# Six units of 512 tokens instead of eight of 384 in a fused attention and two-layer kernel, with the second result kept feature-major

## What is computed

```python
for t in range(S):
    state = alpha[:, :, t, :, None] * state + einsum('bhd,bhe->bhde', k[:, :, t], v[:, :, t])
    y[:, :, t] = einsum('bhd,bhde->bhe', q[:, :, t], state)
```

## Time and profile before

| quantity | value |
|---|---|
| median of 3 runs | 1025.24 us (1024.99 to 1027.24) |
| profiled execution, span | 1023.4 us |
| PE busy | 999.5 us, 98% |
| DVE, ACT, POOL busy | 399.3, 464.0, 81.0 us |
| mean granted PE clock | 0.997 of 2.4 GHz |
| instructions in the span | 16903 |

### The profile page before, as it was taken

How to read it: one execution, slowest core, us unless ns; L and a number is a source line. 1 busy time by engine, 2 the same in 40 slices (tenths; PEclk the granted TensorE clock), 3 DMA queues, 4 the chain that set the end, 5 groups by cost and what they waited for, 6 DMA issues and landing times.

```text
span 1023.4 us, 16903 instructions
## 1 busy us (share of the span) xinstructions
PE 999.5 (98%) x6146; PEld 950.8 (93%) x6146; DVE 399.3 (39%) x805; ACT 464.0 (45%) x1017; POOL 81.0 (8%) x110
## 2 busy tenths in 40 slices
PE   5989999999999999999999999999999999999997
PEld 5788898998898998998989999999999999999997
DVE  6583563562563743743732451212121212221211
ACT  4464563553543643634634774333333333343432
POOL 4663300000000000000000430000000000000000
PEclk9999999999999999999999999999999999999999
DMA  7661340230320321222000531010000000000000
GB/s 169 159 143 49 77 101 13 61 68 18 77 47 18 76 47 38 58 49 44 25 7 18 161 113 37 11 37 21 26 22 25 23 23 24 23 25 21 23 0 26
DMA packets 118465, 51.21 MB, mean 50 GB/s; under 512 B 103040, under 2 KB 115328, under 8 KB 118400
## 3 DMA queue, kind: packets, MB, share of 16 engines
q1 hardware_dynamic: 114304, 37.76, 15.5%
q0 software_dynamic: 4096, 12.59, 3.9%
HBM read 36.18 MB, written 9.44 MB: 45 GB/s over the span
## 4 chain that ended last, share of the span: by engine, by line
PE 95%; DVE 2%; issue 1%; ACT 1%; DMA 1%; SPq 0%; POOL 0%; DVEq 0%; ACTq 0%
PE z_ps L557 40%; PE h_ps L544 39%; PE job_ps L514 4%; PE job_ps L528 3%; PE job_ps L494 3%; PE job_ps L524 3%; PE job_ps L507 2%; PE job_ps L499 1%; DVE qp L814 1%; DVE rcp L819 0%; ACT L717 0%; DMA nat_a<-in_alpha 0%; DMA x_raw<-y_sb 0%; PE h_ps L586 0%; DVE kp L827 0%
## 5 line engine op out<-in xcount | busy, mean ns | idle before, releaser
L884 DVE TENSOR_TENSOR g_lo<-g,g_hi 128x384 fp32r<-128x384 f32 x256 | 141.2, 552 | 573.4 <-ACT g_hi L720 322.3
L544 PE MATMUL h_ps<-x_hi,win_hi 128*128 128x384 f32 x768 | 259.8, 338 | 4.7 <-issue 1.6
L544 PE MATMUL h_ps<-x_hi,win_lo 128*128 128x384 f32 x768 | 258.4, 336 | 0.0
L544 PE MATMUL h_ps<-x_lo,win_hi 128*128 128x384 f32 x768 | 258.4, 336 | 0.0
L717 ACT ACTIVATE g<-h_ps 128x384 f32<-128x384 f32 x128 | 62.9, 492 | 221.7 <-PE h_ps L544 221.6
L723 ACT ACTIVATE relu<-h_ps 128x384 f32<-128x384 f32 x128 | 62.7, 490 | 218.2 <-PE h_ps L544 213.5
L544 PEld LDWEIGHTS h_ps<-x_hi,win_hi 128*128 128x128 f32 x768 | 144.1, 188 | 6.5 <-ACT g L717 2.0
L544 PEld LDWEIGHTS h_ps<-x_lo,win_hi 128*128 128x128 f32 x768 | 144.1, 188 | 0.0
L544 PEld LDWEIGHTS h_ps<-x_hi,win_lo 128*128 128x128 f32 x768 | 144.1, 188 | 0.0
L557 PE MATMUL z_ps<-g_hi,wout_hi 128*128 128x384 f32 x384 | 138.0, 359 | 0.0
L557 PE MATMUL z_ps<-g_hi,wout_lo 128*128 128x384 f32 x384 | 129.5, 337 | 0.0
(11 more groups left out here) (68 smaller groups left out, 1016.7 us busy)
## 6 DMA issues: line engine op xcount, KB each, us to landing
w_raw<-in_moe_w_in POOLq DMA_DIRECT2D x32, 192.0 KB, 3.0
w_raw<-in_moe_w_out POOLq DMA_DIRECT2D x32, 192.0 KB, 2.7
nat_a<-in_alpha SPq DMA_DIRECT2D x24, 192.0 KB, 3.4
nat_k<-in_k SPq DMA_DIRECT2D x24, 192.0 KB, 3.5
nat_q<-in_q SPq DMA_DIRECT2D x24, 192.0 KB, 3.8
v_sb<-in_v SPq DMA_DIRECT2D x24, 192.0 KB, 3.8
z_scratch<-z_sb SPq DMA_DIRECT2D x24, 192.0 KB, 1.9
x_raw<-z_scratch SPq DMA_DIRECT2D x8, 576.0 KB, 4.0
```

The source lines that it names most:

```text
L544: last = nc.tensor.matmul(h_ps[f % 2][:, 0:UT], w[:, f, tile(kk)], x[par][:, kk, :], start=(kk == 0 and n == 0), stop=(kk == KD - 1 and n ...
L884: nc.vector.tensor_tensor(g_lo[s % 3][:], g[s % 2][:], g_hi[s % 3][:].bitcast(F32), ALU.subtract).then_inc(g_lo_made, 1)
```

## The change

The time axis is cut differently. A unit is one chunk of 128 tokens of all four batches: 6 units (UNITS = SEQ // P) of UT = 512 tokens. The products of both layers then have 512 columns; there are 6 x 16 x 18 of them in a layer instead of 8 x 16 x 18.

- The steps of both layers form one line of 192 (F), written out without loops, and the second product is two steps behind the first also across units and from layer one to layer two.
- The second layer's second product has w_out as weights, as the first layer's. Its result is feature-major in PSUM; DVE turns it in blocks of 32x32 (`turn_z`), and w_out's columns are permuted when they are split so that a row of a token's result lies in runs of 96 floats. A unit is stored by 16 DMAs of 48 KB with runs of 384 bytes; those of the last unit are shared by SP and ACT.
- The attention works on 24 pair units n (unit n // 4, pair n % 4; four tiles, one of each batch) in stages: A, KQ, S (scores of both heads, and KT), I, Y. Stages of n = 0 to 3, and A of n = 4, run ahead of everything (AHEAD). Those of n = 4 to 7 take three steps a pair, from n = 8 on four steps a pair. The last four pair units have no KT and I. A is no longer copied by ACT: DVE's scan reads PSUM. nat, kp, qp and v are kept for two pairs, not for a unit.
- Loads bring one head of one pair unit (96 KB) instead of one chunk of all heads (192 KB). 20 chunks of weights are split ahead of the first step instead of 16, five to a pair. The `relu` tile is gone; g is squared in place.

```diff
-UT = 384
-NC = UT // P
-UNITS = TOK // UT
+UNITS = SEQ // P
+UT = BATCH * P
+AHEAD = [("A", 0), ("A", 1), ("KQ", 0), ("S", 0), ("A", 2), ("KQ", 1), ("I", 0), ("Y", 0), ("S", 1), ("A", 3),
+         ("KQ", 2), ("I", 1), ("Y", 1), ("S", 2), ("KQ", 3), ("I", 2), ("Y", 2), ("S", 3), ("I", 3), ("Y", 3), ("A", 4)]
+FIRST_PE = {0: 6, 1: 8, 2: 8, 3: 4}
+WARM_AFTER = 24
+EARLY_CHUNKS = 20
+def stage_step(kind, n):
+    if n < 2 * PAIRS:
+        return {"A": -1, "KQ": 1, "S": 2, "I": 3, "Y": 3}[kind] + 3 * (n - PAIRS)
+    return {"A": -21, "KQ": -19, "S": -18, "I": -17, "Y": -16}[kind] + 4 * n
+    # within a step: S, A, I, Y, KQ
...
 # PE
+            def a_stage(n):
+                loaded("a", n)
+                if n > PAIRS:
+                    if has_state(n - 1):
+                        wait(pe, kt_copied, n)
...
+            def kq_stage(n):
...
+                turn("k", n, job_ps[0]).then_inc(k_made, 1)
+                loaded("q", n)
+                if n > PAIRS and has_state(n - 1):
+                    wait(pe, inc_made, 2 * n)
+                else:
+                    wait(pe, masked, 2 * n - 1)
+                turn("q", n, job_ps[1]).then_inc(q_made, 1)
+            def s_stage(n):
+                wait(pe, k_scaled, n + 1)
+                wait(pe, q_scaled, n + 1)
+                wait(pe, y_copied, n)
+                for b in range(BATCH):
+                    for h in (0, 1):
+                        r = head_rows(h)
+                        last = nc.tensor.matmul(job_ps[1 + h][:, tile(b)], kp[n % 2][r, tile(b)], qp[n % 2][r, tile(b)],
                                                 start=True, stop=True)
...
+            def y_stage(n):
...
+                    for b in range(BATCH):
+                        nc.tensor.matmul(ps[0:ROWS, tile(b)], state[:, p, b, :], qp[n % 2][:, tile(b)],
+                                         start=(b == 0), stop=False, skip_group_check=True)
+                for b in range(BATCH):
+                    for h in (0, 1):
+                        last = nc.tensor.matmul(ps[head_rows(h), tile(b)], v_sb[n % 2][:, b, h, :], score[h][:, b, :],
...
             def first_product(u, par, f, w_hi, w_lo):
                 wait(pe, act_made, NF * u + f - 1)
...
+            for F in range(2 * STEPS + LAG):
+                u, f = divmod(F, NF)
...
+                        first_product(u, u % 2, f, win_hi, win_lo)
+                    for kind, n in beside(F):
+                        stage(kind, n)
...
 # ACT
+            for n in range(PAIRS):
+                bounds(n)
+                for c in range(5 * n, 5 * n + 3):
+                    split_chunk(c)
+                kt_copy(n)
+                for c in range(5 * n + 3, 5 * n + 5):
+                    split_chunk(c)
+                y_copy(n)
+            split_x(0, ys=1)
+            bounds(PAIRS)
+            for F in range(2 * STEPS):
+                u, f = divmod(F, NF)
+                step(u, f, F % 3, u >= UNITS)
+                if u < UNITS:
+                    square_g(f)
+                if u == 0 and EARLY_CHUNKS + f < NCHUNK:
+                    split_chunk(EARLY_CHUNKS + f)
...
+                if f == 1 and 1 <= u <= UNITS:
+                    copy_z(u - 1, u - 1, u - 1)
+                for kind, n in beside(F):
+                    if kind == "S" and has_state(n):
+                        kt_copy(n)
+                    if kind == "Y":
+                        y_copy(n)
+                for kind, n in beside(F - 1):
+                    if kind == "A":
+                        bounds(n)
...
 # DVE
+            def a_stage(n):
+                at, ps = qp[n % 2], a_bank(n)
...
+                for b in range(BATCH):
+                    nc.vector.tensor_tensor_scan(out=at[:, tile(b)], data0=ps[0:ROWS, tile(b)], data1=floor[:],
...
+                for half in (0, 1):
+                    cols = slice(half * UT // 2, (half + 1) * UT // 2)
+                    nc.vector.reciprocal(rcp[:, cols], at[:, cols]).then_inc(rcp_made, 1)
...
+            def turn_z(parted, stored):
...
+                    nc.vector.transpose(z_turned_sb[:, :, m, :], z_ps[m][:].rearrange("p (c t) -> p c t", t=32)
+                                        ).then_inc(z_turned, 1)
...
+            for n in range(PAIRS):
+                if n == 0:
+                    a_stage(0)
+                    kq_stage(0)
+                else:
+                    a_stage(n)
+                    s_stage(n - 1)
+                    kq_stage(n)
+            s_stage(PAIRS - 1)
+            for n in range(PAIRS):
+                i_stage(n)
+                state_stage(n)
+            split_x(0, 0)
+            a_stage(PAIRS)
```

More of the change, by code:

```diff
@@ L156, in repack_pieces, with has_state, beside @@
+BESIDE = {}
+for _n in range(PAIRS, LASTP + 1):
+    for _k in ("S", "A", "I", "Y", "KQ"):
+        BESIDE.setdefault(stage_step(_k, _n), []).append((_k, _n))
+def has_state(n):
+    return n <= LASTP - PAIRS
+def beside(step):
+    jobs = BESIDE.get(step, []) if isinstance(step, int) and step >= 0 else []
+    return sorted((j for j in jobs if j[0] != "I" or has_state(j[1])), key=lambda j: ("S", "A", "I", "Y", "KQ").index(j[0]))
 def repack_pieces(pair):
@@ L700, in split_x, with y_slot_free, bounds @@
-            def split_x(u, par, ys=None, zs=None):
+            def y_slot_free(units, p):
+                wait(act, y_moved[p % 2], moved(units, p))
+            def bounds(n):
+                wait(act, rcp_made, 2 * (n + 1))
+                nc.scalar.activation(square[:], qp[n % 2][:], ACT.Square, accum_out=bound[:, n, 0:1]).then_inc(bound_made, 1)
+                wait(act, bound_made, 2 * n + 1)
+                nc.scalar.activation(square[:], rcp[:], ACT.Square, accum_out=bound[:, n, 1:2]).then_inc(bound_made, 1)
+                wait(act, bound_made, 2 * n + 2)
@@ L875, in split_x @@
                                             ALU.subtract).then_inc(x_lo_made, 1)
-            def unit(u, par, second, at1=None, at2=None, chunks=None, split=True, skipped=0):
-                for s in range(NF):
-                    F = NF * u + s
-                    G = F - NF * skipped
-                    if not second:
-                        wait(dve, g_made, G + 1)
-                    wait(dve, g_hi_made, F + 1)
-                    nc.vector.tensor_tensor(g_lo[s % 3][:], g[s % 2][:], g_hi[s % 3][:].bitcast(F32),
-                                            ALU.subtract).then_inc(g_lo_made, 1)
-                    for n in chunks(s) if chunks else ():
-                        split_w(n, *chunk(n)[:2], n + 1)
-                    if s == SPLIT_STEP and split:
-                        split_x(u + 1, 1 - par)
-                    attention(s, at1, at2)
```

920 lines of the change are left out of this document (425 added, 495 removed), and 4 rows, old and new, of the table AHEAD1.

## The result

The kernel after takes 989.85 us (median of 4 runs, 987.58 to 992.49) against 1025.51 us of the kernel before beside it: a ratio of 0.9652, 95% interval 0.9634 to 0.967, so 35.7 us faster. The profiled execution has a span of 988.1 us, where the prediction's sum was 983.4.

The account below looks back on a forecast made before the run. PE's row of matmuls was taken to bound the kernel, plus head and tail. Head 60, products 783.4, attention 112, stalls 12.5, delays 5.5, last product 0.4 and tail 9.6 gave 983.4 us of span, 985 us in all; range 955 to 1004.

Parts of the forecast that it names:

- the products' pace: Both layers' products: 3456 matmuls of 512 columns at 226.7 ns, 783.4 us against 798.7 before, -15.3 us.
- the attention's matmuls: PE's attention stages for twenty pair units beside the products: 5.8 us each, 112 us in all, -44 us.
- small delays: Both layers together: 5.5 us kept for small delays, with turns of the hardware loops and doubled products at units' ends gone.
- head: Stretch up to the first product: 60 us (57 to 66), +9.0, with part possibly at the lower clock.
- stalls in unit 0, clock included: PE waits for ACT and DVE in unit 0: 10.8 us in sum, taken as 12.5 with the clock (0 to 18).
- last product's way: End of the last product, between products and tail: 0.4 us of the span.
- tail: Behind the last product, one DVE turn, eight stores each on SP and ACT, flight: 9.6 us (8 to 12), +4.5.
- a fixed cost: Products: the 13.3 ns above the columns' time belongs to each matmul, so 226.7 ns at 512 columns.
- the share: Rival on the products: the excess is a share of the columns, 231.1 ns a matmul, 1000 us; chance 0.18.
- The rival of the dear wide matmul: Products: 512-column matmuls cost more; at 238.3 ns the gain is gone, at 245 the kernel takes 1048 us; chance 0.04.
- DVE's chain: Head: q's scaling for four pairs, then scores, masks, four state updates and x_lo, ending at 57.9 us.
- y's: Head, parallel chain: POOL's chunks, chunk 19 ahead of y_copy(3), two moves by SP, x_hi and x_lo, ending at 58.5 us.

Follow-up runs that it names:

- the run with 256 columns: Changed kernel with some first products of unit 5 and the second layer cut in columns, weights or depth; at 256 columns starts were 120 ns apart in unit 5.
- Both undoings: Two runs against the changed kernel: stage Y tile by tile again, 1008.61 us; stage S one head after the other, 1005.45 us.
- either fix of a visible stall in unit 0: Two runs against the changed kernel: ACT's bounds(4) moved behind step 0, 988.21 us; ACT's copy of turned kp ahead of squares and chunk, 989.64 us.

## Why the prediction was right

The forecast was 985 us, the median 989.85; of the span, 983.4 against 988.1. What carried it were the products' pace and the attention's matmuls, which make up all of the gain, and both came out as reasoned. Two smaller terms, the small delays and the head, hold errors that the total hides. Term by term, in us:

| term | forecast | measured | from |
|---|---|---|---|
| head | 60 | 61.87 | windows |
| 3456 products at 226.7 ns | 783.4 | 783.4 | first layer's intervals |
| attention of 20 pair units | 112 | 111.6 | step lengths over 4.08: 87.6 in units 1 to 5, and 24.0 in unit 0 at the same prices |
| stalls in unit 0, clock included | 12.5 | 13.4 | what is left of the first layer's 512.65 |
| small delays | 5.5 | 6.4 | second layer |
| last product's way | 0.4 | 0.2 | windows |
| tail | 9.6 | 11.3 | windows |
| span | 983.4 | 988.1 | |

- **Products.** The choice of a fixed cost held at 512 columns, and the run with 256 columns shows it at a third width. It rested on 13.3 ns being 32 cycles, which was an argument, not a row; the chance of 0.18 for the share was fair to that. The Trainium skill ("TensorE: Matmul & The Clock Gate", "Back-to-back issue gap") gives N/2.4 + 2.5 ns as the gap of an isolated matmul, and for a stream of weight loads and matmuls a sustained pace of about 131 ns at 512 columns. The prediction read the first as a rule for such a stream, which the section does not say; the 226.7 ns of this case agree with neither figure.
- **Attention.** Right in sum and nearly by stage: S with KT 1.66 (1.6), Y 2.15 (2.1), A with KQ and I 2.19 (2.1). Both undoings price their part: grouping Y is worth 19 us, interleaving S 11. Of the 44 us of the forecast's gain some 7 moved ahead of the first product; 19 and up to 11 are these two (before, some scores of two heads already stood together); what is left, 7 us or more by this estimate, no run isolates. Two slips of the sum are small: KT and I of four pair units are 4.8 us by its own prices and not 4, and 12 transposes at 0.1 with two changes are 1.4 and not 1.3. In the steps with attention the second products start some 231 ns apart instead of 226.7, and the table counts that as attention. What made this sizing possible were the rows of the same instructions in other company, six and twelve scores, one tile of Y.
- **Stalls.** Places and causes as forecast: 2.9 us ahead of the third first product (3.6 forecast); at steps 5, 8 and 11 PE's weight load is idle for 1.36 us and PE itself for 1.18 (1.5 forecast). At step 2 the kernel lost 2.6 where 1.2 and 1.5 were given. With 1.36 that makes 9.6 of the 13.4; the rest is the lower clock and what I can't tell from it. In the kernel after, PE ran at 1.2 GHz for 3.4 us behind the 2.9 of idle (window: length, busy times, clock):

```profile
71.20:74.60 3.40, 3.40 (x19) 2.55 (x19) 2.42 (x4) 3.34 (x8) 2.50 (x3) 0.50 0.02 5
```

- **Small delays.** The number was right for a wrong reason. I kept 5.5 us for unit ends and for delays in both layers. There were none at unit ends or in units 1 to 5; all 6.4 us were the misaligned weights of the second layer. The rival of the dear wide matmul had named the sign of it, operands in other places, and its price was 7 ns, not 25. Its evidence was read too broadly: the mean of 176.0 ns in the second layer of before holds unit ends beside the 3.3 ns of its first products. That the term fits is luck.
- **Head.** 1.9 too low, and with the wrong chain last. Fourth scaling at 48.05 against 47.4, and from there to the first product 13.8 against 12.6. The forecast had DVE's chain end at 57.9, y's at 58.5, and took 60 for the lower clock. PE did run at the lower clock in part of this stretch (16 matmuls of pair 3's Y in 1.95 us, 1.08 at full clock), but y was not last: x_lo stood behind DVE's state updates and ended its first tile at 61.6. They had been priced at 7 us for four and took 9.6; 2.7 of it are the three multiplications beside POOL's subtractions. The scores and masks took 3.3 instead of 2.8, and the first product came 0.26 behind x_lo, directly behind the last matmul of `keep_warm`.
- **Tail.** 1.7 too low in this execution, 0.8 to 1.3 in the ten other kernels that store on two queues: 0.66 us a store on SP and 0.73 on ACT instead of 0.6, and 4.7 us of flight and end instead of 3.9. Before, from the end of the last issue to the end it had been 4.1.

The tail's error is one of issue and flight of small moves, priced at the mean of a range of rows and not at its upper end. The head's is a row taken from one place, where its engine had been little disturbed, and used in another where POOL worked beside it.

## What to carry to other kernels

Price an instruction by its fixed cost and its columns from two widths before widening tiles: the gain is the number of instructions saved by the fixed part. Group matmuls by operand shape and alternate those that use different partitions: here 0.16 us for each change of shape and 0.55 for eight pairs side by side. And look at the start address of every matmul operand: small tensors put ahead of large ones shift them, and a pad of 32 bytes was worth 6.4 us, more than either fix of a visible stall in unit 0. A stall that two chains hold up together goes only when both are shortened.

## What the runs showed of the hardware

- An fp32r matmul whose loaded or streamed operand starts 32 bytes past a multiple of 64 took 233 ns for 512 columns, against 226.7 with both at a multiple. At 256 columns no such cost was seen (117 ns with misaligned weights, 120 without).
- The excess over the columns' time was 13.3 ns at 256, 384 and 512 columns, where equal matmuls followed one another.
- In the kernel after, DVE's 40 multiplications of the state (48x192 numbers, both inputs in SBUF) took 0.82 to 1.75 us in the six cases where a subtraction by POOL overlapped them, and at most 0.36 in the 34 others. In every other kernel of these runs, the one before included, each overlapped one took longer (0.38 us at least) than any that was not overlapped (0.36 at most).
- The attention's fp32 matmuls and DVE and ACT passes showed no such effect: with their buffers moved to multiples of 64 the steps of units 1 to 4 changed by 0.03 us at most, and in sum by nothing.
- POOL issued stores at 0.55 us each beside SP's 0.66 and ACT's 0.66.
